# First pair's values: load on ScalarE's queue, sum on VectorE, spread ahead of the first scores

## The reference, cut to what matters

```python
k_sum = k.reshape(B, H, nb, 32, D).max(axis=3)      # 24 key maxima
v_sum = v.reshape(B, H, nb, 32, D).mean(axis=3)     # 24 value means
scores_l = scale * q @ k.T, masked to |i - j| < 16
scores_s = scale * q @ k_sum.T + log(32)
a = softmax(concat(scores_l, scores_s))
attn = a @ concat(v, v_sum)
# then a token mixing layer (256 wide), a channel mixing layer (1536 wide),
# a layer norm and a second channel mixing layer (2048 wide), all on [2, 768, 512]
```

## Time and profile before

| | us |
|---|---|
| median of 3 runs | 611.28 (610.35 to 612.75) |
| profiled execution, device time | 612.84 |
| its span, first to last instruction | 611.1 |
| TensorE busy in the span | 594.0 (97%) |
| VectorE, ScalarE, GpSimd busy | 219.8, 159.4, 49.6 |
| mean granted TensorE clock | 0.994 of full |

### The profile page before, as it was taken

How to read it: one execution, slowest core, us unless ns; L and a number is a source line. 1 busy time by engine, 2 the same in 40 slices (tenths; PEclk the granted TensorE clock), 3 DMA queues, 4 the chain that set the end, 5 groups by cost and what they waited for, 6 DMA issues and landing times.

```text
span 611.1 us, 7428 instructions
## 1 busy us (share of the span) xinstructions
PE 594.0 (97%) x2808; PEld 484.1 (79%) x2808; DVE 219.8 (36%) x537; ACT 159.4 (26%) x331; POOL 49.6 (8%) x91
## 2 busy tenths in 40 slices
PE   6899999999999999999999999999999999999997
PEld 2677888878888788878888788888788888788886
DVE  5387666466334311134533632112521113211112
ACT  3376664334323101113332310112111102101110
POOL 5356541000000000000000000000000000000000
PEclk9799999999999999999999999999999999999999
DMA  8877532014333000000223100000100000100001
GB/s 231 226 210 225 168 106 96 17 35 137 104 104 104 1 0 1 0 1 8 96 103 104 34 2 2 0 1 0 70 0 1 0 1 0 70 1 0 1 0 69
DMA packets 21305, 35.58 MB, mean 58 GB/s; under 512 B 7596, under 2 KB 7832, under 8 KB 21272
## 3 DMA queue, kind: packets, MB, share of 16 engines
q1 hardware_dynamic: 20720, 34.69, 18.5%
q10 hardware_dynamic: 552, 0.44, 0.3%
HBM read 31.39 MB, written 3.15 MB: 57 GB/s over the span
## 4 chain that ended last, share of the span: by engine, by line
PE 92%; DVE 3%; issue 2%; DMA 2%; ACT 1%; POOL 0%; SPq 0%; DVEq 0%; ACTq 0%; POOLq 0%
PE bank L367 88%; PE bank L516 1%; DMA k_sb<-k_w 1%; DVE neg_scores L725 1%; DMA v_far<-v_mean 1%; PE bank L400 1%; PE bank L402 1%; PE bank L401 1%; DVE k_sb L713 1%; ACT probs L594 0%; DVE natural L844 0%; POOL v_tree L328 0%; ACT tok_w L610 0%; DVE x_split L707 0%; DVE natural L738 0%
## 5 line engine op out<-in xcount | busy, mean ns | idle before, releaser
L820 DVE SCALAR_TENSOR_TENSOR hidden<-bank,hidden 128x512 fp32r<-128x512 f32 x84 | 58.1, 691 | 309.3 <-ACT hidden L644 309.3
L367 PE MATMUL bank<-slots_late,hidden 128*128 128x512 f32 x648 | 156.4, 391 | 0.0
L644 ACT ACTIVATE hidden<-bank 128x512 fp32r<-128x512 f32 x84 | 50.2, 598 | 353.7 <-PE bank L367 353.7
L367 PEld LDWEIGHTS bank<-slots_late,hidden 128*128 128x128 f32 x648 | 120.9, 188 | 24.7
L367 PE MATMUL bank<-in_t,slots_late 128*128 128x512 f32 x576 | 137.7, 389 | 1.1 <-issue 1.1
L367 PEld LDWEIGHTS bank<-in_t,slots_late 128*128 128x128 f32 x576 | 107.9, 188 | 24.5 <-issue 2.3
L367 PE MATMUL bank<-in_t,slots_early 128*128 128x512 f32 x288 | 69.5, 390 | 0.0
L367 PEld LDWEIGHTS bank<-in_t,slots_early 128*128 128x128 f32 x288 | 54.1, 188 | 11.7
L367 PE MATMUL bank<-slots_early,hidden 128*128 128x512 f32 x216 | 51.9, 389 | 0.0
L367 PEld LDWEIGHTS bank<-slots_early,hidden 128*128 128x128 f32 x216 | 40.5, 188 | 8.4
L367 PE MATMUL bank<-k_sb,q_sb 128*128 128x364 f32 x96 | 39.7, 499 | 4.2 <-DVE neg_max L725 2.5
(11 more groups left out here) (72 smaller groups left out, 430.0 us busy)
## 6 DMA issues: line engine op xcount, KB each, us to landing
stage<-w_ch SPq DMA_DIRECT2D x56, 256.0 KB, 2.7
k_sb<-k_w SPq DMA_DIRECT2D x16, 273.0 KB, 4.2
v_own<-v_w SPq DMA_DIRECT2D x8, 390.0 KB, 3.1
q_sb<-q_t SPq DMA_DIRECT2D x8, 384.0 KB, 4.9
v_turned<-v_t SPq DMA_DIRECT2D x8, 384.0 KB, 3.7
out<-natural SPq DMA_DIRECT2D x12, 256.0 KB, 2.1
tok_stage<-w_tok SPq DMA_DIRECT2D x4, 384.0 KB, 4.0
v_far<-v_edge SPq DMA_DIRECT2D x16, 45.0 KB, 2.9
```

The source lines that it names most:

```text
L367: return nc.tensor.matmul(dst, lhs, rhs, start=start, stop=stop, skip_group_check=True)
L644: nc.scalar.activation(hidden[:, f % HID_RING, 0, :], ch1_bank[f % 2][:, 0:GN], ACT.Relu).then_inc(hid_high, 1)
L820: nc.vector.scalar_tensor_tensor(out=hidden[:, f % HID_RING, 1, :], in0=ch1_bank[f % 2][:, 0:GN], scalar=0.0, in1=hidden[:, f % HID_RING, ...
```

## The change

- The turned values of pair 0 are loaded as the first transfer of ScalarE's queue and no longer by SyncE. The identity comes second, then the mask, then ones, then the gain.
- VectorE sums them (one reduction, 768 elements of each partition to 24), between the first and the other two of its clears of the keys; the memset of `v_sum` is now its second instruction. GpSimd no longer sums pair 0; its first sum is that of pair 1.
- TensorE makes 13 warm products, turns the sums, waits for the copy of the means, and makes 6 more warm products ahead of the first scores. ScalarE copies the means and issues their spread itself, ahead of the first exponentials.
- `v_init` and the fill of `v_far` are gone. The edges come from memory as whole rows with their ones and zeros (3120 bytes), and two transfers `value_ones` put 48 such rows in place of the means' rows, once for each buffer. The spread of pair 0's means waits for both.
- SyncE's loads of values 0 and 1 wait for nothing now, and the spread of pair 0's means no longer stands in its queue.

```diff
-WARM = 16
+WARM = (13, 6)
...
+        def send_means(queue, r):
+            i = r % 2
+            queue.wait_ge(mean_copied, r + 1)
+            if r >= 2:
+                queue.wait_ge(pv_done, NT * (r - 1))
+            else:
+                queue.wait_ge(ld_ones, 32)
+            for h in range(2):
+                at = SUM_ROW[h]
+                queue.dma_start(v_far[at:at + NSUM, i, :, 1 + h * D:1 + (h + 1) * D],
+                                v_mean[:, i, h * D:(h + 1) * D].rearrange("p (t n) -> p t n", t=1)
+                                .broadcast_to([NSUM, NT, D])).then_inc(ld_mean[i], 16)
...
                 if r >= 2:
                     sp.wait_ge(pv_done, NT * (r - 1))
-                else:
-                    sp.wait_ge(far_init, r + 1)
                 sp.dma_start(v_own[:, i], v_w[b, p]).then_inc(ld_v[i], 16)
                 for h in range(2):
-                    sp.dma_start(v_far[EDGE_ROW[h]:EDGE_ROW[h] + TAIL, i, :, 1 + h * D:1 + (h + 1) * D],
+                    sp.dma_start(v_far[EDGE_ROW[h]:EDGE_ROW[h] + TAIL, i],
                                  v_edge[b, p, h]).then_inc(ld_edge[i], 16)
...
             load_k(0)
             load_q(0)
-            load_turned(0)
             load_v(0)
             load_turned(1)
             load_k(1)
             load_q(1)
-            send_means(0)
             load_v(1)
...
             spread_keys(0)
-            sum_values(0)
             sum_values(1)
...
             pe.wait_ge(warm_ready, 1)
-            for _ in range(WARM):
+            for _ in range(WARM[0]):
+                mm(mix_bank[:], warm[:, 0:P], warm[:], True, True)
+            pe.wait_ge(ld_ident, 16)
+            pe.wait_ge(init_done, 3)
+            turn_sums(0, mix_bank[:, mean_at])
+            pe.wait_ge(mean_copied, 1)
+            for _ in range(WARM[1]):
                 mm(mix_bank[:], warm[:, 0:P], warm[:], True, True)
             pe.wait_ge(k_clear, CLEARS)
             scores(0)
             scores(1)
             scores(2)
-            pe.wait_ge(ld_ident, 16)
-            pe.wait_ge(init_done, 3)
-            turn_sums(0, mix_bank[:, mean_at])
             turn(0)
...
-            act.dma_start(v_init[:], value_init).then_inc(ld_init, 16)
+            act.dma_start(v_turned[:, 0, :], v_t[0, 0]).then_inc(ld_vt[0], 16)
+            act.dma_start(ident[:], identity).then_inc(ld_ident, 16)
             act.dma_start(mask_sb[:], mask).then_inc(ld_mask, 16)
-            act.dma_start(ident[:], identity).then_inc(ld_ident, 16)
+            for i in range(2):
+                act.dma_start(v_far[TAIL:TAIL + 2 * NSUM, i], value_ones).then_inc(ld_ones, 16)
             act.dma_start(gain_sb[:], gain).then_inc(ld_gain, 16)
+            copy_means(0, mix_bank[0:NSUM, mean_at])
+            send_means(act, 0)
             exps(0)
             exps(1)
-            copy_means(0, mix_bank[0:NSUM, mean_at])
...
             dve.sem_inc(w_split, STAGES)
-            for i in range(KB):
-                clear_keys(nc.vector, 0, i)
+            nc.vector.memset(v_sum[:], 0.0).then_inc(init_done, 1)
             for i in range(2):
                 nc.vector.memset(turn_bank[i][96:P, P:2 * P], 0.0).then_inc(init_done, 1)
-            nc.vector.memset(v_sum[:], 0.0).then_inc(init_done, 1)
-            dve.wait_ge(ld_init, 16)
-            for i in range(2):
-                nc.vector.tensor_copy(v_far[:, i], v_init[:].rearrange("p (t v) -> p t v", t=1)
-                                      .broadcast_to([2 * NB, NT, PV])).then_inc(far_init, 1)
+            clear_keys(nc.vector, 0, 0)
+            dve.wait_ge(ld_vt[0], 16)
+            dve.wait_ge(init_done, 1)
+            nc.vector.tensor_reduce(v_sum[:, 0, 0:NSUM], v_turned[:, 0, :].rearrange("p (n s) -> p n s", s=BLOCK),
+                                    AX_X, ALU.add).then_inc(vsum_done, 1)
+            for i in range(1, KB):
+                clear_keys(nc.vector, 0, i)
             for h in range(2):
                 key_maxima(0, h)
```

More of the change, by code:

```diff
@@ L66, in build @@
 def build(nc, q_t, k_w, v_w, v_edge, v_t, w_tok1, w_tok2, w_ch1, w_ch2, w2_ch1, w2_ch2, gain, mask,
-          value_init, identity, out):
+          value_ones, identity, out):
     ctx = ExitStack()
@@ L97, in build @@
             v_mean = sb(a, "v_mean", [NSUM, 2, P])
-            v_init = sb(a, "v_init", [2 * NB, PV])
             neg_scores = sb(a, "neg_scores", [P, 2, 2, NK])
@@ L125, in build @@
         ld_gain = sem("ld_gain")
-        ld_init = sem("ld_init")
-        far_init = sem("far_init")
+        ld_ones = sem("ld_ones")
         ld_k = [sem(f"ld_k{i}") for i in range(KB)]
@@ L283, in _ @@
                 if r + 1 < NPAIR:
-                    send_means(r + 1)
+                    send_means(sp, r + 1)
                 if r + KB < NPAIR:
@@ L332, in sum_values @@
                         op.then_inc(tree_step, 1)
-                        pool.wait_ge(tree_step, 4 * r + j + 1)
+                        pool.wait_ge(tree_step, 4 * (r - 1) + j + 1)
                         src, lo = v_tree[:, :, lo:lo + n], lo + n
@@ L915, in constants @@
         mask[:, kind, NSUM:NSUM + WIN] = np.where(there, 0.0, MASKED / SCALE)
[L916 to L919, removed]
+    value_ones = np.zeros((2 * NSUM, NT, PV), np.float32)
+    value_ones[0:NSUM, :, 0] = 1.0
+    value_ones[NSUM:, :, PV - 1] = 1.0
+    return mask, value_ones, np.eye(P, dtype=np.float32)
 def kernel(q, k, v, moe_w_tok1, moe_w_tok2, moe_w_ch1, moe_w_ch2, moe2_g_ln, moe2_w_ch1, moe2_w_ch2):
@@ L925 @@
     from concourse.bass_utils import run_bass_kernel_spmd as _run
-    mask, value_init, identity = constants()
+    mask, value_ones, identity = constants()
     def turned(a):
@@ L942, in value_windows @@
         own = np.ones((B, PAIRS, P, NT, PV), a.dtype)
-        edge = np.zeros((B, PAIRS, 2, TAIL, NT, D), a.dtype)
+        edge = np.zeros((B, PAIRS, 2, TAIL, NT, PV), a.dtype)
+        for h in range(2):
+            edge[:, :, h, :, :, h * (PV - 1)] = 1.0
         for t in range(NT):
@@ L946, in value_windows @@
                 own[:, :, :, t, 1 + h * D:1 + (h + 1) * D] = a[:, :, h, t * P + mine:t * P + mine + P]
-                edge[:, :, h, :, t, :] = a[:, :, h, t * P + rest:t * P + rest + TAIL]
+                edge[:, :, h, :, t, 1 + h * D:1 + (h + 1) * D] = a[:, :, h, t * P + rest:t * P + rest + TAIL]
         return own, edge
@@ L963 @@
         "gain": np.ascontiguousarray(np.asarray(moe2_g_ln).reshape(C, P).T),
-        "mask": mask, "value_init": value_init, "identity": identity,
+        "mask": mask, "value_ones": value_ones, "identity": identity,
     }
```

## The result

The change made the kernel slower: 617.85 us (616.99 to 619.78, 7 runs) against 611.85 (610.35 to 614.38, 7 runs), ratio 1.0098 with a 95% interval of 1.0076 to 1.0119. I had forecast 606.3 in a range of 604.0 to 609.3.

The account below looks back on a forecast made before the run. TensorE was taken as bound early by the means' landing and the low clock. Gains of 3.2 (weighting) and 2.9 (clock) less 0.3 (start-up) gave 5.8; less 0.8 for the median, 5.0: 606.3 us, range 604.0 to 609.3.

Parts of the forecast that it names:

- What bounds the kernel now: At the start, TensorE's first weighting waits 4.32 us for the means in v_far, then runs at low clock.
- Landing of the turned values: Pair 0's turned values, first on ScalarE's queue, land at 5.5 us, bounds 4.4 and 6.9.
- What it displaces on VectorE: Clears and key maxima stand behind the wait for turned values; scores come at 11.1, 1.9 us later than before.
- From the scores to the products: Exponentials, turning and copy after the scores make probs_t ready at 14.7 us.
- The means' own path: Sums turned, copied, then spread behind the ones; means land at 14.6, first weighting at 14.9, a gain of 3.2 us.
- My part on the loads: SyncE's queue no longer waits and edges grow to 91 KB; keys 1 land at 11 to 15; cost nothing.
- The clock: TensorE's longest early idle time is 2.1 us, so the clock stays up: tiles 0 and 1 gain 2.9 us.
- Start-up: A smaller stock of scores and probabilities at the first weighting, with VectorE busy in tiles 0 and 1: 0.3 us charged.
- (a): The means' small pieces take turns with SyncE's large ones and land at 16.2, giving 607.9 us; chance 0.13.
- (b): The clock falls anyway in TensorE's idle time ahead of the scores, giving 608.9 us; chance 0.10.
- (d): Turned values land late behind SyncE's transfers, delaying clears, maxima and scores; at 12, 614.6 us; chance 0.05.
- (c): Loads bound pair 1 or 2 and take back TensorE's lead, giving 609.5 to 611.3 us; chance 0.10.

Follow-up runs that it names:

- run 6: The changed kernel with pair 0's means as whole rows holding their own ones, sent by SyncE directly behind values 0; ratio 1.0002, 611.2 us.
- run 9: The kernel before with only pair 0's turned values first on ScalarE's queue, VectorE's reduction and divided warm products, timed again; ratio 0.9996, 611.43 us.
- run 1: The changed kernel with pair 0's means spread from SyncE's queue again, behind queries 1; ratio 1.0023, 613.1 us.
- run 5: The changed kernel with pair 0's means sent by ScalarE as whole rows, without the first ones transfer or the wait for ones; ratio 1.0000, 611.29 us.
- run 4: The changed kernel with 32 more warm products between turning 1 and the first weighting; ratio 1.0086, 616.61 us.
- the reordered kernel: Run 9's kernel with the means behind turned values 1 in SyncE's queue and the identity ahead of v_init; ratio 1.0010.

## Why the prediction was wrong

- **What bounds the kernel now** was right for the first tile and too narrow. The landing of the means did end the last wait at 18.09. But right behind it stood other waits, for loads that must be there by tile 6, which the chain of waits can't show while TensorE is late. Run 6 removed the first bound whole and came out level.
- **Landing of the turned values**: forecast 5.5 (4.4 to 6.9), measured 4.15. **The reduction**: 0.95, as forecast.
- **What it displaces on VectorE**: scores forecast at 11.1, measured 10.78. The right size for another reason. The maxima waited for keys 0 (second half landed at 8.1, 6.7 before) and TensorE for queries 0 (10.65, 7.7 before). ScalarE's now longer queue moved beside them, and it wasn't in my reckoning of them at all. What slowed them wasn't taken apart; in run 9 (one part of the change alone, the second time), with the turned values on ScalarE's queue but neither ones nor early loads of values 0, queries 0 landed at 8.7.
- **From the scores to the products**: forecast 14.7, measured 15.8. I had passed over the gain, now last in ScalarE's queue: it landed at 13.4, and VectorE's masks stood before it, behind a wait that I had not listed (idle 3.40, of which the wait for the scores would have taken a part: 1.75 before).
- **The means' own path** is the step that failed. Ones: forecast 9.5, measured 11.53, inside the bounds of 8.5 and 14. Two issues: 2.25 instead of 1.78. Landing: forecast 4.19, bounds 2.9 and 7.4, measured 10.17. The error was to carry over a duration from another queue and another load. In the kernel before, SyncE waited for the means before it issued more, and by their issue all but 0.4 MB ahead of them had moved; the change took this wait away, and 3.2 of the 5.2 MB issued had still to move. My part on the loads had written that the wait was gone, and cost it at nothing; it had keys 1 down at 11 to 15, and they landed at 17.3. Ones, issues and landing together are 8.6 us, against the 8.5 by which the first weighting missed its 14.9.
- **The clock**: forecast to stay up, it fell. With the landing at 23.2 that follows. But run 1 says more: it fell there too, with 2.64 us as the longest idle time. It fell in run 5 with 2.35, and stayed up in run 9 with 2.36 at the same place; in run 6 it stayed up behind 2.42 and fell behind 2.27. The length of the longest idle stretch, by which I had judged, doesn't tell. The term's size, 2.9, was right (3.1 in run 4).
- **Start-up** (0.3) and **TensorE keeps what it has behind tile 3**: the second is shown, with a delay of 5.5 from tile 3 to the end. The first was not measured by itself.
- **Rivals**: (a), at 0.13, was the mechanism of the second part, with half of its price: a lag of about 4 us with no packet moving, and over 5 us of turns, where I had 2.9 and 2.9. My one argument against it, the 4.19 behind a whole backlog, had misread its row: only 0.4 MB were left ahead of the means there. (b) didn't come where I had it: 2.41 us idle ahead of the scores left the clock at 1.00. (d), which I had made the slower case, named another place. (c) would have decided had the means been in time: run 6.
- **The range.** The forecast's own range, 604.6 to 607.6, doesn't follow from its two terms: the values at 5.0 with a clock's part of 2.9 give 605.0, the values at 6.0 give 606.8. Nothing of the outcome hangs on it.
- What stays open: what the lag of 4 us is, and how much of the lead of run 6 goes to loads, and how much to the pace of VectorE and ScalarE.

## What to carry to other kernels

A wait in a queue that issues transfers is also a throttle: before it is taken away, write down how many bytes go out past it, and what small transfer will have to land beside them. Price a transfer by a row with the same neighbours, not by one with the same shape; and list every wait on the last transfer of a queue that grows, the small ones too. Before a chain is shortened by some us, ask which load would be late if the engine were that much ahead, since the chain of waits shows only the latest of several bounds.

## What the runs showed of the hardware that I had not expected

- A transfer on ScalarE's queue stood for about 4 us without a packet while SyncE's queue held the 16 engines at 103%, in the form of 288 pieces and of 48 rows alike, and landed 7.4 to 7.5 us behind its second issue (rows, issued at 9 us as at 13 us) or 10.2 (pieces). With 2.3 MB less in SyncE's queue it still stood 3.4 us, and 4.2 in SyncE's queue itself.
- ScalarE's queue got 0.35 of the first 0.6 MB from 2 to 4 us, so with large rows in both the two queues shared about evenly there; from 17 to 23 us, with 256-byte pieces, it got 0.07 of 1.56.
- A load of v_init of 54.8 KB took 4.3 us when issued second on ScalarE's queue, at 1.17 (run 9), and 7.1 when issued third, at 1.66, with 64 KB more ahead of it (the reordered kernel).
